# Fused FFT and two MLPs on one core: first weights loaded in pieces, x folded by units, first inverse norm moved forward

## The reference

```python
X = np.fft.fft(np.fft.fft(x, axis=1), axis=2).real       # x: 2 x 3008 x 256
t = X.reshape(6016, 256)
tn = t / np.sqrt(np.mean(t * t, -1, keepdims=True) + 1e-6) * rms_g
h = silu(tn @ w_gate) * (tn @ w_val)                      # 1536 wide
y = h @ w_out                                             # 256 wide
out = (g * np.cos(g)) @ w2_out,  g = y @ w2_in            # 2048 wide
```

## Time and profile before

| | |
|---|---|
| three timed runs | 992.68, 993.01, 999.22 us; median 993.01 |
| profiled execution | 993.36 us |
| its span, first to last instruction | 991.6 us |
| PE busy | 979.0 us of the span |
| DVE, ACT, POOL busy | 740.9, 644.5, 352.1 us |

### The profile page before, as it was taken

How to read it: one execution, slowest core, us unless ns; L and a number is a source line. 1 busy time by engine, 2 the same in 40 slices (tenths; PEclk the granted TensorE clock), 3 DMA queues, 4 the chain that set the end, 5 groups by cost and what they waited for, 6 DMA issues and landing times.

```text
span 991.6 us, 12885 instructions
## 1 busy us (share of the span) xinstructions
PE 979.0 (99%) x4452; PEld 810.0 (82%) x4452; DVE 740.9 (75%) x1024; ACT 644.5 (65%) x804; POOL 352.1 (36%) x294
## 2 busy tenths in 40 slices
PE   7999999999999999999999999999999999999998
PEld 7877878888888888888888888888888888888886
DVE  6768888768877768877667887767887767887665
ACT  3688768775358775448775348776348776437777
POOL 0179676007750007751006661004771003771000
PEclk9999999999999999999999999999999999999999
DMA  9858310001010001000001010001000000100001
GB/s 313 264 133 236 107 32 11 1 1 42 1 33 11 1 1 42 1 31 10 0 0 41 0 31 11 0 0 41 1 15 17 0 0 0 42 0 0 0 0 42
DMA packets 12480, 37.46 MB, mean 38 GB/s; under 512 B 2520, under 2 KB 6488, under 8 KB 11800
## 3 DMA queue, kind: packets, MB, share of 16 engines
q1 hardware_dynamic: 10364, 32.30, 9.6%
q0 software_dynamic: 2064, 4.72, 2.6%
q10 hardware_dynamic: 12, 0.00, 0.0%
HBM read 23.02 MB, written 9.26 MB: 33 GB/s over the span
## 4 chain that ended last, share of the span: by engine, by line
PE 94%; DMA 2%; ACT 1%; issue 1%; SPq 1%; DVE 1%; POOL 0%; ACTq 0%; DVEq 0%
PE ps L505 30%; PE ps L506 30%; PE ps L507 30%; DMA seq<-t_seq 2%; PE ps L464 1%; PE ps L481 1%; SPq L305 1%; PE ps L479 0%; PE ps L493 0%; ACT uv L621 0%; POOL work L1128 0%; DVE work L986 0%; ACT w_hi L675 0%; ACT squares L651 0%; DVE h_lo L921 0%
## 5 line engine op out<-in xcount | busy, mean ns | idle before, releaser
L505 PE MATMUL ps<-h_hi,wo_hi 128*128 128x502 f32 x672 | 262.1, 390 | 1.2 <-DVE h_lo L921 1.2
L507 PE MATMUL ps<-h_hi,wo_lo 128*128 128x502 f32 x672 | 261.5, 389 | 0.0
L506 PE MATMUL ps<-h_lo,wo_hi 128*128 128x502 f32 x672 | 261.4, 389 | 0.0
L1037 POOL TENSOR_TENSOR h_lo<-work,h_hi 128x502 fp32r<-128x502 f32 x92 | 102.4, 1120 | 375.7 <-ACT h_hi L739 372.5
L724 ACT ACTIVATE h_hi<-work 128x502 fp32r<-128x502 f32 x132 | 82.6, 626 | 174.3 <-POOL work L1128 174.3
L1024 DVE SCALAR_TENSOR_TENSOR work<-work,ps 128x1004 f32<-128x1004 f32 (+1 forms) x109 | 117.2, 1075 | 95.1 <-ACT work L819 94.6
L1010 DVE SCALAR_TENSOR_TENSOR work<-work,ps 128x1004 f32<-128x1004 f32 (+1 forms) x109 | 116.4, 1073 | 48.6 <-ACT work L805 48.6
L505 PEld LDWEIGHTS ps<-h_hi,wo_hi 128*128 128x128 f32 x672 | 126.4, 188 | 29.5 <-issue 1.6
L505 PE MATMUL ps<-x_hi,win_hi 128*128 128x502 f32 x384 | 149.9, 390 | 0.0
L506 PE MATMUL ps<-x_lo,win_hi 128*128 128x502 f32 x384 | 149.3, 389 | 0.0
L507 PE MATMUL ps<-x_hi,win_lo 128*128 128x502 f32 x384 | 149.2, 389 | 0.0
(11 more groups left out here) (86 smaller groups left out, 1286.1 us busy)
## 6 DMA issues: line engine op xcount, KB each, us to landing
out<-y_sb SPq DMA_DIRECT2D x10, 502.0 KB, 3.1
x_sb<-x SPq DMA_DIRECT2D x6, 768.0 KB, 11.2
w_lo<-w_f POOLq DMA_DIRECT2D x6, 512.0 KB, 6.2
uv_t<-uv_dram SPq DMA_DIRECT2D x6, 502.0 KB, 3.5
wo_raw<-wo SPq DMA_DIRECT2D x1, 2048.0 KB, 10.0
win_raw<-win SPq DMA_DIRECT2D x1, 2048.0 KB, 9.8
raw_b<-w1b SPq DMA_DIRECT2D x1, 1536.0 KB, 19.1
raw_a<-w1a SPq DMA_DIRECT2D x1, 1536.0 KB, 23.1
```

Source lines behind the costliest of these rows:

```text
L505: nc.tensor.matmul(acc, w_hi, v_hi, start=start, stop=False)
L506: nc.tensor.matmul(acc, w_hi, v_lo, start=False, stop=False)
L507: return nc.tensor.matmul(acc, w_lo, v_hi, start=False, stop=stop)
L1037: nc.gpsimd.tensor_tensor(dst, src, hi.bitcast(F32), ALU.subtract).then_inc(s, 1)
```

## The change

- `CHUNKS` becomes [1, 1, 1, 3, 3, 3, 3, 3, 3, 2, 1], `HALF_FOLDED` (3, 5, 10): units 1 and 2 are chunks of their own, and seven units in place of four get only the addition. In stage 1 PE takes the two outputs c of a unit one after the other, no longer all units of a group for c = 0 and then for c = 1.
- The negative half of `t_seq1` is no longer loaded; ACT makes it on chip at its start.
- `t_seq2` comes in rows 0 to 3, 4 to 9, 10 to 16; behind each part a third of `raw_b` and of `raw_a` (two column blocks, 2 KB rows), with semaphores of their own.
- `SCALE_AT`, `MIX_AT`, `W1_SPLIT_AT` move to earlier steps.
- `rms(1)` and `rms(6)` come one step sooner, `sequence` of the last steps one step later, `root(0)` ahead of the copy of pair 5 (it was behind pair 6), `add_epsilon(0)` at step 13 (14), `recip(0)` at step 14 (16), `split_uv(0)` at pair 11 (12), `square(8)` behind the first Silu, `rms(8)` in the third `up1`.
- The means of parts 0 and 1 are spread by SP, around `store_uv(0)`, no longer by ACT.
- POOL's list is put in another order: `inverse(0)` behind `add_squares(2)`, `scale_uv(0)` ahead of `w1_add(3)` and `add_squares(5)`.

```diff
-CHUNKS = [1, 2, 3, 3, 3, 3, 3, 3, 2, 1]
-HALF_FOLDED = (4, 9)
+CHUNKS = [1, 1, 1, 3, 3, 3, 3, 3, 3, 2, 1]
+HALF_FOLDED = (3, 5, 10)
...
-        RMS_AT = [8, 10, 15, 20, 23, 27, 32]
+        RMS_AT = [8, 9, 15, 20, 23, 27, 31]
...
-        SCALE_AT = [3, 4, 5, 6, 7, 10]
-        MIX_AT = [8, 9, 11, 12, 15, 17, 19, 21, 23, 25, 27, 29]
-        W1_SPLIT_AT = {5: 0, 7: 1, 11: 2, 15: 3}
+        SCALE_AT = [2, 3, 6, 7, 12, 16]
+        MIX_AT = [4, 5, 8, 9, 10, 11, 15, 17, 22, 24, 26, 28]
+        W1_SPLIT_AT = {3: 0, 5: 1, 7: 2, 9: 3}
...
+        SEQ2_PARTS = [slice(0, 4), slice(4, 10), slice(10, K1)]
...
-            load(seq1[:, :], t_seq1, seq1_in)
+            load(seq1[:, 0:COLS1], t_seq1, seq1_in)
...
-            load_seq2(slice(0, SEQ2_FIRST), seq2_in)
-            load(raw_b[:, :], w1b, raw_b_in)
-            load(raw_a[:, :], w1a, raw_a_in)
-            load_seq2(slice(SEQ2_FIRST, K1), seq2_rest)
+            def load_raw(dst, src, i, s):
+                part = lambda w: w.rearrange("p (m n c) -> p m n c", m=2, n=3)[:, :, i, :]
+                load(part(dst), part(src), s)
+
+            for i in range(3):
+                load_seq2(SEQ2_PARTS[i], seq2_in[i])
+                load_raw(raw_b[:, :], w1b, i, raw_b_in[i])
+                load_raw(raw_a[:, :], w1a, i, raw_a_in[i])
...
+            spread_mean(0)
             store_uv(0, (slice(0, 1), slice(1, FIRST_ROWS)))
+            spread_mean(1)
...
             for G in range(LAST):
                 features(G)
-                if G >= 2:
+                if 2 <= G < LAST - 3:
                     sequence(G - 2)
+                if G >= LAST - 2:
+                    sequence(G - 3)
                 if G in RMS_AT:
                     rms(RMS_AT.index(G))
-            sequence(LAST - 2)
+            sequence(LAST - 3)
...
+            act.wait_ge(seq1_in, 16)
+            nc.scalar.activation(seq1[:, COLS1:2 * COLS1], seq1[:, 0:COLS1], ACT.Copy, scale=-1.0
+                                 ).then_inc(seq1_negated, 1)
...
-                if q < ACT_MEANS:
-                    act.wait_ge(mean_out, q + 1)
-                    act.dma_start(stat[stat_rows(*PART_ROWS[q]), 0, :], mean_row[:, q % ROWS, 0:z - a]
-                                  ).then_inc(mean_in[q], 16)
...
             for p in range(LAST // 2):
+                if p == 5:
+                    root(0)
                 uv_copy(p)
                 row0_copy(p)
...
+                if p == 11:
+                    split_uv(0)
                 split_step(p)
-                if p == 6:
-                    root(0)
...
-                if p == 12:
-                    split_uv(0)
...
                     if first and i == 0:
+                        square(MEANS - 1)
                         for q in RMS_LATE:
                             mean_copy(q)
...
+                if G == 13:
+                    add_epsilon(0)
                 if G == 14:
-                    add_epsilon(0)
-                if G == 16:
                     recip(0)
...
-            for q in range(3):
-                add_squares(q)
+            add_squares(0)
+            add_squares(1)
             w1_add(0)
+            add_squares(2)
+            inverse(0)
+            w1_add(1)
             add_squares(3)
-            w1_add(1)
-            inverse(0)
+            w1_add(2)
             add_squares(4)
+            scale_uv(0)
+            w1_add(3)
             add_squares(5)
-            scale_uv(0)
             scale_u128(0)
-            w1_add(2)
-            add_squares(6)
...
             last.then_inc(uv_split, 1)
+            add_squares(6)
             wo1_add(0)
             add_squares(7)
-            w1_add(3)
             add_squares(8)
```

More of the change, by code:

```diff
@@ L51, in tables @@
     seq1 = seq1.reshape(P, -1)
-    seq1 = np.concatenate([seq1, -seq1], axis=1)
     d = np.arange(P)
@@ L74, in tables @@
     f = lambda v, c: np.ascontiguousarray(v.reshape(v.shape[0], c), dtype=np.float32)
-    return {"t_seq1": f(seq1, 4 * BATCH * 2 * K1), "t_feat": f(feat, FEAT + DIM),
+    return {"t_seq1": f(seq1, 2 * BATCH * 2 * K1), "t_feat": f(feat, FEAT + DIM),
             "t_seq2": f(seq2, K1 * 2 * N2), "t_const": f(const, 2)}
@@ L176, in build @@
         x_in = [sem(f"x_in{i}") for i in range(XL)]
[L177 to L182, removed]
+        seq1_in, feat_in, const_in, small_in = (sem(n) for n in ("seq1_in", "feat_in", "const_in", "small_in"))
+        seq2_in = [sem(f"seq2_in{i}") for i in range(3)]
+        wo1_in, win2_in, wo2_in = (sem(n) for n in ("wo1_in", "win2_in", "wo2_in"))
+        raw_a_in, raw_b_in = ([sem(f"raw_{ab}_in{i}") for i in range(3)] for ab in "ab")
+        even_done, odd_done, folded, n1_done, n1_out, seq1_negated = (sem(n) for n in (
+            "even_done", "odd_done", "folded", "n1_done", "n1_out", "seq1_negated"))
         pq_done, pq_out, uv_done, uv_main, uv_row0 = (sem(n) for n in (
@@ L230, in part_end @@
             return b * STEPS + k.stop - 1
-        RMS_AT = [8, 10, 15, 20, 23, 27, 32]
+        RMS_AT = [8, 9, 15, 20, 23, 27, 31]
         MEAN_COPY_AT = [2, 3, 7, 9, 11, 13, 15]
-        ACT_MEANS = 2
         RMS_LATE = range(len(RMS_AT), MEANS)
@@ L263, in build @@
         FIRST_ROWS = 6
-        SEQ2_FIRST = 10
+        SEQ2_PARTS = [slice(0, 4), slice(4, 10), slice(10, K1)]
         UV_FIRST, UV_BATCH, UV_ALL = 32, 64, 112
@@ L435, in _ @@
             for g, ms in enumerate(GROUPS):
[L436 to L443, removed]
+                for i, m in enumerate(ms):
+                    if m in CHUNK_AT:
+                        if m:
+                            warm_up(2 if CHUNK_AT.index(m) < 4 else 0)
+                        pe.wait_ge(folded, CHUNK_AT.index(m) + 1)
+                        if CHUNK_AT.index(m) == HALF_FOLDED[0]:
+                            pe.wait_ge(seq1_negated, 1)
+                    for c in range(2):
+                        if i == 0 and g >= 2:
+                            pe.wait_ge(n1_out, 2 * (g - 2) + c + 1)
                         acc = ps[:, (2 * g + c) % 4, i * COLS1:(i + 1) * COLS1]
@@ L452, in _ @@
                                                     start=True, stop=True)
-                    last.then_inc(n1_done, 1)
+                        if i == len(ms) - 1:
+                            last.then_inc(n1_done, 1)
             pe.wait_ge(n1_out, 2 * NG)
             pe.wait_ge(feat_in, 16)
-            pe.wait_ge(seq2_in, 16)
+            pe.wait_ge(seq2_in[0], 16)
             def features(G):
@@ L475, in sequence @@
                     pe.wait_ge(uv_row0, 2 * (G // 2 - 1))
-                if G == SEQ2_FIRST:
-                    pe.wait_ge(seq2_rest, 16)
+                for i in (1, 2):
+                    if G == SEQ2_PARTS[i].start:
+                        pe.wait_ge(seq2_in[i], 16)
                 bank = 4 + G % 4
@@ L573, in tile @@
                 up1(t, 1, halves=(1,))
-                if first:
-                    rms(RMS_LATE[1])
                 if not first:
@@ L578, in tile @@
                 for i in range(2, C1):
-                    up1(t, i)
+                    up1(t, i, halves=(0,))
+                    if first and i == 2:
+                        rms(RMS_LATE[1])
+                    up1(t, i, halves=(1,))
                     if first and i == 2:
@@ L593, in _ @@
             up1(0, 0, halves=(0,))
+            sequence(LAST - 2)
             sequence(LAST - 1)
@@ L706, in _ @@
                 for q in parts_ending(p):
-                    square(q)
+                    if q < MEANS - 1:
+                        square(q)
                 for q in means_copied(p):
                     mean_copy(q)
+                if p == 11:
+                    split_uv(0)
                 split_step(p)
-                if p == 6:
-                    root(0)
                 if p == 14:
                     root(1)
-                if p == 12:
-                    split_uv(0)
             def hi1(t, i):
@@ L887, in split_step @@
                 if G in SCALE_AT:
-                    if G == SCALE_AT[0]:
-                        dve.wait_ge(raw_b_in, 16)
+                    dve.wait_ge(raw_b_in[SCALE_AT.index(G) // 2], 16)
                     n = W1_ORDER[SCALE_AT.index(G)]
@@ L898, in split_step @@
                     dve.wait_ge(scaled_b, k // 2 + 1)
-                    if k == 0:
-                        dve.wait_ge(raw_a_in, 16)
+                    if k % 4 == 0:
+                        dve.wait_ge(raw_a_in[k // 4], 16)
                     if k // 2 >= SLOTS:
```

## The result

The changed kernel took 999.06 us (median of 22 runs, 997.26 to 1001.42), the kernel before in the same series 996.76 (22 runs, 992.68 to 1001.34): ratio 1.0031, interval 1.0017 to 1.0045. The medians differ by 2.3 us and the means by 3.1, as the ratio does. The forecast was 994.3, slower by 1.3: the direction was right, the size not. It also started too low: from the median of three runs of the kernel before, 993.01, where 22 give 996.76. Each run also records its mean granted clock of PE, and that turned out to matter. All 22 runs of the changed kernel had 0.997 or 0.998. Of the 89 runs of the kernel before that were made beside the experiments, 31 had 1.000, at 993.4 us on average; those with 0.998 took 995.6 to 996.5 (averages by series).

What follows compares the result with a forecast made beforehand. PE, busy 99%, bounds the kernel; only time ahead of D counts. 65.4 + 14.2 + 1.5 put D at 81.1, 1.3 us later: 993.36 + 1.3 = 994.7 profiled, median 994.3, range 990.8 to 997.2 (8 in 10).

Steps and rivals of the forecast that it cites:

- What bounds the kernel: Whole kernel: PE busy 979.0 of 991.6 us, at most 12.6 us to gain; only time ahead of D can change.
- D: PE's first `down` matmul, at 79.82 us before, forecast 81.1; the end moves by whatever it moves by.
- Stage 1: Start of kernel: first `features` at 26.2, a gain of 0.2 us (0 to 0.5), which disappears in later waits.
- The means, L: Landing of the mean rows of parts 0 and 1, held on SP's queue behind `wo1_raw` and `store_uv(0)`: 42.5 (40.0 to 43.3).
- The chain from L to `store_inv`: Steps on DVE and ACT from epsilon to `mean_copy(2)`, 6.4 us, then SP's `spread_mean(2)`, 0.46: L + 6.86.
- From `store_inv` at 53.42 to `scale_uv(0)` at 59.08 it took 5.66: The inverse's trip through DRAM, duration taken from the profile before; with it POOL scales at L + 12.5.
- POOL: [...] 10.0: POOL's list from `scale_uv(0)` through `add_squares(6)`, durations summed to 10.0 us.
- So `rms(6)` starts at L + 22.9: Stage 2, PE: `rms(6)` at 65.4 for L = 42.5, against 65.65 before.
- The clock: PE in stage 1: levels 1.2 and 2.4 GHz; six more matmuls cost 1.5 us at the upper, 3.2 at the lower.
- It waits 3.9 us in sum, in front of `sequence(14)`, `sequence(16)` and several `rms`: PE's waits up to `rms(6)`: own work would end at 61.5, so 3.9 us of waiting, which swallows stage 1's gain.
- From `rms(6)` to D: 14.17 us as before plus 1.5 for three more pieces of step work; D's own 0.96 wait stays (-0.3 to +0.5).
- Rival B: Raw blocks in 2 KB rows keep SP's queue busy longer: D at 87.1, 7.3 us later, 1000.3 us; chance 0.10.

Runs made afterwards that it cites:

- fill_wait: Changed kernel with 18 spare matmuls of 128 columns on PE ahead of `rms(5)`, filling its wait: 996.69 us, ratio 1.0018 to the kernel before.
- add2_late: Changed kernel with POOL's `w1_add(2)` moved behind `scale_uv(0)`: 999.07 us, ratio 1.0038 to the kernel before.
- adds_late: Changed kernel with POOL's `w1_add(1)` and `w1_add(2)` both moved behind `scale_uv(0)`: 1000.37 us in one execution.
- sq5_first: Changed kernel with POOL's `add_squares(5)` back ahead of `scale_uv(0)`: 997.74 us, ratio 1.0035 to the kernel before.
- combo_tail: The kernel of `combo` with `square(8)` and `rms(8)` back at their places of the kernel before: 993.17 us, ratio 0.9985 to the kernel before.
- combo: Changed kernel with the `wo1_raw` load behind `load_inv(0)` and POOL's list reordered, `add_squares(5)` ahead of `scale_uv(0)`: 994.15 us, ratio 1.0004 to the kernel before.
- the last one: The kernel of `combo_tail` with `rms(6)` back at step 32: 991.46 us, ratio 0.9936 to the kernel before; on another chip 991.66 us, ratio 0.9957.

## Why the prediction was wrong

Point by point, by the prediction's own steps:

- *What bounds the kernel* was right: everything happened ahead of D, and what lies behind it did not change.
- *Stage 1* was right in result: the first `features` at 25.91 (forecast 26.2), ACT's last copy as the next to be late, the gain swallowed by later waits, 0.42 us at `sequence(14)` and 0.61 at `sequence(16)` first, both named by the prediction. Stage 1 by itself was not settled.
- *The means, L.* The value was right (42.67 against 42.5), partly by luck, and the reason was not. ACT's own queue gives 42.48 in the same place. I read the trace of before as a queue that overtakes; it only showed a row that landed by 41.98. The store that the row stood right behind was no bound either: it was issued after 36.0 and took 7.0 us, so it landed at 43.0 or later, behind epsilon. What the runs show is that `wo1_raw` in flight keeps the row back: with it moved away epsilon came at 40.21, right behind the step that it belongs to. The rule of the Trainium skill that I weighed (DMA: Bandwidth & Descriptors, queues, rings and completion order), as I applied it, would have had the row from ACT overtake; the measurement decides, and here it was used 0.2 us sooner, no more. L also varies: 40.95 to 43.05 in five profiles with the same steps up to there (the changed kernel's, `fill_wait`, `add2_late`, `adds_late`, `sq5_first`), so one profile of each kernel does not resolve half a microsecond.
- *The chain from L to `store_inv`* was right to 0.02 us.
- *"From `store_inv` at 53.42 to `scale_uv(0)` at 59.08 it took 5.66"* is the first term that failed. It was carried over to a place where a weight addition had 3.2 us still to come instead of 1.3, with a second one behind it, and measured 8.79. Without them it is 5.08. `scale_uv(0)` came 3.3 us later than the forecast of L + 12.5 for L = 42.5.
- *"POOL: [...] 10.0"* was too long. From the start of `scale_uv(0)` at 58.30 to the end of `add_squares(6)` at 66.80 it was 8.5, partly since the sum adds the whole 2.7 us of the subtraction into `uv_lo` where the next instruction starts 2.2 us after it. This hid half of the error before it.
- *"So `rms(6)` starts at L + 22.9"* took the wrong wait as the last one. With `scale_uv(0)` at 58.30, `rms(5)` behind `add_squares(5)` was, at 62.69. My list had `add_squares(5)` in this place, and I named `rms(5)` among those that would wait, but I did not ask from which landing on it would bind PE. `rms(6)` then ran without a wait, at 68.59 (forecast 65.4), 1.8 us behind the end of `add_squares(6)`.
- *The clock* is the term that I put at nothing behind stage 1. *"It waits 3.9 us in sum, in front of `sequence(14)`, `sequence(16)` and several `rms`"* missed that most of it would come in one piece, and that such a piece costs more than its length. PE's idle stretch from 58.4 to 62.7 was followed by the 1.2 GHz level. Filling the wait gave back 2.4 us.
- *From `rms(6)` to D* I had 14.2 + 1.5 = 15.7; it was 16.5, at a full clock too. D's own wait was forecast as unchanged within -0.3 to +0.5; it rose from 0.96 to 1.37. That the places of `square(8)` and `rms(8)` cost something is shown by `combo_tail` against `combo`, 1.1 us at equal clock.

Put together: the time was 4.8 us over the forecast of 994.3. Of this, 2.4 are the clock, put at nothing; 2.0 are the delay at a full clock, 3.3 instead of 1.3, which come from the mis-sized trip and the order behind it (`combo`, with another order and an earlier landing, takes 2.6 of the 3.3 away); 0.4 are the start from 993.01, where the runs at a full clock average 993.4. The difference to the kernel before is smaller than 3.3 + 2.4, because that kernel loses 2.6 us to the clock itself (its 89 runs beside the experiments average 996.0, those at a full clock 993.4). Against each other the two clocks nearly cancel; that is luck, not something that I had foreseen. Rival B (2 KB rows) did not happen: `wo1_raw` landed 16.6 us after 25.34, at 41.94, 0.6 us later than before.

## What to carry to other kernels

In this kernel a DMA's time from issue to use depended on what was in flight beside it. When a step is moved, take its duration again from the traffic at its new place, and for a small round trip among weight loads ask how much of the transfer ahead of it is still to come. List, for an engine with a fixed order, what each waiting consumer needs, and look for the first that binds, not for the last; putting work that needs no DMA ahead of work that does brought more here than a shorter trip. On a PE-bound kernel a wait can cost more than its length. The kernel whose longest wait in stage 2 is 4.25 us lost clock in 22 of 22 runs, the kernel before (1.59 us) in 58 of 89, the last one (0.70 us) in none of 17. Look at the granted clock behind a wait, and compare runs of equal clock before calling a difference the edit's. A median of three runs can hide this: 993.01 became 996.76 with 22.

## What the runs showed of the hardware that was not expected

- The kernel before, unchanged, runs at 993.4 us on average at a full clock and at 993.8 to 1002.0 us in the 58 runs under it; the share of runs at a clock of 1.000 was 10 of 27, 15 of 29, 1 of 17 and 5 of 16 in four series. A kernel without long waits in stage 2 had 17 of 17. Why the chips differ is open.
- An issue of two small DMAs on SP took 2.05 us beside accumulating DMAs (0.62 before, 0.76 with them moved away).
- Small rows that SP stored to DRAM beside a 512 KB accumulating DMA came when it did: in ten profiles the load that waits for them was issued 0.0 to 0.4 us behind its landing, up to 4.3 us behind the store. Without one in flight it was 1.7.
- Two mean rows issued by different engines at 36.99 and 37.52 were used at 42.67 and 42.48: an engine's own queue gave little or no lead.
